# Third pair normalised in place, and a shorter way from the last token chunk to the first expert tile

## The reference

```python
mag = np.sqrt(a_re * a_re + a_im * a_im)
scale = np.minimum(mag, 0.999) / (mag + 1e-06)
a_re_n, a_im_n = (a_re * scale, a_im * scale)
for t in range(S):                                   # 768 steps
    new_re = ar * S_re - ai * S_im                   # state D x D, D = 48
    new_im = ar * S_im + ai * S_re
    S_re, S_im = (new_re + outer(k[t], v[t]), new_im)
    y[t] = q[t] @ S_re
```

```python
logits = xn @ en.T / tau
expert_idx = np.argmax(logits, axis=1)
for e in range(E):
    mask = expert_idx == e
    out[mask] = gate_w[mask, None] * (np.maximum(x[mask] @ w1[e], 0.0) @ w2[e])
```

## Time and profile before

| | |
|---|---|
| median of 3 runs | 994.85 us (993.94 to 995.58) |
| the profiled execution, its own time | 994.46 us |
| its span | 992.7 us |
| PE (TensorE matmul) busy | 872.8 us, 88% |
| DVE (VectorE) busy | 658.2 us, 66% |
| POOL (GpSimd) busy | 495.0 us, 50% |
| ACT (ScalarE) busy | 462.5 us, 47% |

### The profile page before, as it was taken

One profiled execution on the slowest core, in us unless ns is written; L12 is line 12 of the kernel. 1 busy time (PEld: TensorE's weight loads), 2 busy tenths in 40 slices (PEclk: granted clock), 3 DMA queues, 4 the chain that ended last, 5 costly groups with the idle time before them and its releaser, 6 DMA issues.

```text
span 992.7 us, 18419 instructions
## 1 busy us (share of the span) xinstructions
PE 872.8 (88%) x6398; PEld 776.7 (78%) x6399; DVE 658.2 (66%) x1054; ACT 462.5 (47%) x859; POOL 495.0 (50%) x888
## 2 busy tenths in 40 slices
PE   1658888788989998999999999839999999999995
PEld 1446777687879888889889888838888888888785
DVE  5967876789798998999876755167323252556722
ACT  4776734555646566565344441133222242446521
POOL 1291999699977978889791000023222232323221
PEclk9968997999999999999999999967999999999998
DMA  9104241352424243231311110334411141406311
GB/s 303 62 19 124 79 118 38 77 138 83 113 68 103 69 122 92 82 85 55 86 60 42 38 45 19 138 137 159 175 39 41 40 167 40 166 32 210 122 40 32
DMA packets 42247, 90.80 MB, mean 91 GB/s; under 512 B 6312, under 2 KB 23728, under 8 KB 40768
## 3 DMA queue, kind: packets, MB, share of 16 engines
q1 hardware_dynamic: 38080, 77.48, 25.7%
q0 software_dynamic: 4096, 12.40, 4.0%
HBM read 70.20 MB, written 18.48 MB: 89 GB/s over the span
## 4 chain that ended last, share of the span: by engine, by line
PE 55%; DVE 19%; issue 8%; ACT 8%; DMA 4%; POOL 4%; SPq 1%; DVEq 0%; ACTq 0%; POOLq 0%
PE mm L1582 7%; PE mm L1586 6%; PE mm L1583 6%; PE yu L1582 4%; PE tr L1582 4%; PE tr L1586 4%; PE tr L1583 4%; PE yu L1583 4%; PE yu L1586 4%; PE mm L1820 3%; PE sc L1639 2%; DVE l_im L1094 2%; DVE l_re L1093 2%; PE yu L1680 2%; DVE h_sb L1113 1%
## 5 line engine op out<-in xcount | busy, mean ns | idle before, releaser
L1582 PE MATMUL mm<-up_hi,x_hi 128*128 128x384 f32 x432 | 160.1, 371 | 41.0 <-DVE h_sb L1113 28.9
L1583 PE MATMUL mm<-up_lo,x_hi 128*128 128x384 f32 x432 | 150.7, 349 | 0.0
L1900 POOL TENSOR_TENSOR c_re<-ring 112x128 f32<-112x128 f32 x165 | 99.0, 600 | 102.2 <-DMA ring<-an_scratch 54.0
L1582 PEld LDWEIGHTS mm<-up_hi,x_hi 128*128 128x128 f32 x432 | 83.5, 193 | 57.1 <-DVE h_sb L1113 32.4
L1978 POOL DMA_INDIRECT out_rows<-g_o,rows_out x30 | 34.6, 1155 | 181.7 <-DVE g_o L1499 181.7
L1901 POOL TENSOR_TENSOR c_im<-ring 112x128 f32<-112x128 f32 x165 | 117.9, 714 | 0.0
L956 ACT ACTIVATE g_h<-tr 128x512 f32<-128x512 f32 x60 | 35.9, 598 | 171.2 <-PE tr L1586 165.7
L1586 PE MATMUL mm<-up_hi,x_lo 128*128 128x384 f32 x432 | 103.8, 350 | 0.0
L1904 POOL TENSOR_TENSOR ring<-c_re,c_im 112x64 f32<-112x64 f32 x165 | 91.7, 556 | 0.0
L1903 POOL TENSOR_TENSOR ring<-c_re,c_im 112x64 f32<-112x64 f32 x165 | 80.3, 487 | 12.9
L1113 DVE TENSOR_TENSOR h_sb<-mm,h_sb 128x384 f32<-128x384 f32 x96 | 53.0, 552 | 49.8 <-PE mm L1586 47.9
(11 more groups left out here) (242 smaller groups left out, 2091.4 us busy)
## 6 DMA issues: line engine op xcount, KB each, us to landing
raw<-in_moe_w SPq DMA_DIRECT2D x16, 1536.0 KB
a_dn<-in_a_laid SPq DMA_DIRECT2D x20, 384.0 KB, 6.9
an_scratch<-a_dn SPq DMA_DIRECT2D x20, 384.0 KB, 2.3
ring<-an_scratch SPq DMA_DIRECT2D x20, 384.0 KB, 5.5
q_in<-in_q_laid SPq DMA_DIRECT2D x24, 224.0 KB, 3.0
k_in<-in_k_laid SPq DMA_DIRECT2D x24, 224.0 KB, 3.1
v_in<-in_v_laid SPq DMA_DIRECT2D x24, 192.0 KB, 3.3
x_scratch<-x_sb SPq DMA_DIRECT2D x24, 192.0 KB, 2.1
```

What stands on the lines that cost most here:

```text
L1582: nc.tensor.matmul(out, hi[:, x, :], w_hi(x), start=(x == 0), stop=False)
L1583: nc.tensor.matmul(out, hi[:, x, :], w_lo(x), start=False, stop=False)
L1900: nc.gpsimd.tensor_tensor(c_re[:, 0:count, :, :], cur, bc(prev[:, :, 0, :], 2, 2), ALU.mult).then_inc(chain_prod, 1)
```

## The change

It has two groups of edits.

In the loop: `DIRECT` becomes 3, so pair 2 (units 4 and 5) is loaded straight into `ring` and normalised there, and its two stores and its read back are gone; units 6 to 9 are loaded at the start. The joins of pair 3 move: one behind the decay in turn 4, two early in turn 5, where `stage_z` now stands late. `norm_mag` of a turn's first unit moves ahead of `moe_out` and of `z_recip` on ScalarE, and `norm_sum` of its second unit moves behind `z_newton` and a `moe_max` on VectorE. In `moe_out` the copy of the router columns comes first.

In the routing: VectorE no longer waits for the last store of the tokens, and begins when the last router columns are there. The steps that only the gates need move behind the one-hot matrices, on all engines. The constants are written by GpSimd two chunks sooner (they get memory of their own for it). `row_hot` of the first six chunks is written ahead of `token_hot`. `gate_hot` moves from GpSimd to VectorE. VectorE writes the row lists of the first two gathers itself. The 24 steps of the gates' product (`gates`) move on TensorE between the first and the second matrix of the first tile, and what VectorE makes of them (`tables`) into the first tile. ScalarE starts to split expert 0 two pieces sooner, without the wait for the stores.

```diff
-DIRECT = 2
+DIRECT = 3
...
         joins_early = {1: [(1, b) for b in range(NBLK - 1)]}
         joins_late = {}
         joins_late[2] = [(2, 0)]
         joins_early[3] = [(2, 1), (2, 2)]
-        for g in range(3, NG):
+        joins_late[4] = [(3, 0)]
+        joins_early[5] = [(3, 1), (3, 2)]
+        for g in range(4, NG):
...
+            load_first(4)
+            load_first(5)
...
-                    store_unit(4)
-                    store_unit(5)
                 if n in ring_at:
                     load_ring(ring_at[n])
-                if n == 0:
-                    load_unit(8)
-                    load_unit(9)
...
+                nc.scalar.activation(z_all[:, at, :].rearrange("p t e -> p (t e)"), mm[:, 1, HD:NX], ACT.Copy) \
+                    .then_inc(x2_taken, 1)
...
-                late_z = n in (1, 3)
+                late_z = n in (1, 3, 5)
...
                     norm_rsqrt(4, norm_of(4))
                 if prev:
                     moe_copy(n - 1, 0)
+                for m in norms[:1]:
+                    norm_mag(m, norm_of(m))
                 if prev2:
...
-                for m in norms:
+                for m in norms[1:]:
...
-            act.wait_ge(x2_stored, 16 * NC)
-            for n in range(PIECES):
+            split_hi(0, 0, 0)
+            split_hi(0, 0, 1)
+            act.wait_ge(route_dve, 2)
+            nc.scalar.activation(r_tmp[:, :, :], logit[:, :, :], ACT.Exp).then_inc(route_act, 1)
+            for n in range(2, PIECES):
...
-                for m in norms:
+                for m in norms[:1]:
                     norm_sum(m, norm_of(m))
                 if more:
                     z_newton(n + 1)
                 if prev:
                     moe_max(n - 1, 0, 2)
+                for m in norms[1:]:
+                    norm_sum(m, norm_of(m))
...
-            dve.wait_ge(x2_taken, 2 * NC)
-            dve.wait_ge(x2_stored, 16 * NC)
-            nc.vector.tensor_scalar(nrm[:, 0, :], ssq_all[:, :], TINY, None, ALU.max).then_inc(route_dve, 1)
+            dve.wait_ge(x2_taken, 2 * NC - 1)
...
-            dve.wait_ge(route_act, 2)
-
-            squared = step(nc.vector.tensor_tensor(nrm[:, 3, :], nrm[:, 2, :], nrm[:, 2, :], ALU.mult))
+            dve.wait_ge(x2_taken, 2 * NC)
+            nc.vector.tensor_scalar(nrm[:, 0, :], ssq_all[:, :], TINY, None, ALU.max).then_inc(route_dve, 1)
             after(preferred)
             found = step(nc.vector.tensor_reduce(first[:, :], pick[:, :, :], AX.X, ALU.max))
-            after(squared)
-            newton = step(nc.vector.scalar_tensor_tensor(nrm[:, 4, :], nrm[:, 0, :], -0.5, nrm[:, 3, :], ALU.mult, ALU.mult))
             after(found)
             nc.vector.tensor_tensor(hot[:, :, :].rearrange("p e t -> p t e"), pick[:, :, :], bc(first[:, :], 2, E), ALU.is_equal) \
                 .then_inc(hot_made, 1)
+            dve.wait_ge(route_act, 2)
+            squared = step(nc.vector.tensor_tensor(nrm[:, 3, :], nrm[:, 2, :], nrm[:, 2, :], ALU.mult))
+            after(squared)
+            newton = step(nc.vector.scalar_tensor_tensor(nrm[:, 4, :], nrm[:, 0, :], -0.5, nrm[:, 3, :], ALU.mult, ALU.mult))
...
+            within = step(nc.vector.scalar_tensor_tensor(dest_at[:, 2, :], dest_at[:, 1, :], -float(P), dest[:, :], ALU.mult, ALU.add))
+
             nc.vector.tensor_tensor(in_slot[:, :, :], bc(dest_at[:, 1, :], 2, SLOTS), bc(slot_no[:, :], 1, NC), ALU.is_equal) \
                 .then_inc(in_slots, 1)
+            after(within)
+            nc.vector.tensor_tensor(row_hot[:, 0:CB, :], bc(dest_at[:, 2, 0:CB], 2, P), bc(row_no[:, :], 1, CB), ALU.is_equal).then_inc(rows_hot, 1)
             dve.wait_ge(in_slots, 1)
             nc.vector.tensor_tensor(token_hot[:, :, :], in_slot[:, :, :], bc(token_no[:, :], 2, SLOTS), ALU.mult) \
                 .then_inc(tokens_hot, 1)
-            for part in range(0, NC, CB):
+            for part in range(CB, NC, CB):
                 nc.vector.tensor_tensor(row_hot[:, part:part + CB, :], bc(dest_at[:, 2, part:part + CB], 2, P),
                                         bc(row_no[:, :], 1, CB), ALU.is_equal).then_inc(rows_hot, 1)
 
+            dve.wait_ge(route_act, 3)
+            total = step(nc.vector.tensor_reduce(gate[:, 0, :], r_tmp[:, :, :], AX.X, ALU.add))
+            step(nc.vector.tensor_copy(tiles_i[:, 0, :], bounds[:, 0:E]))
+            after(total)
+            guarded = step(nc.vector.tensor_scalar(gate[:, 1, :], gate[:, 0, :], 1e-9, None, ALU.add))
+            nc.vector.tensor_copy(tiles_i[:, 1, :], bounds[:, 1:E + 1]).then_inc(tiles_ready, 1)
+            after(guarded)
+            gated = step(nc.vector.reciprocal(gate[:, 0, :], gate[:, 1, :]))
+            after(gated)
+            high = step(nc.vector.tensor_copy(gate_parts[:, 0, :], gate[:, 0, :]))
+
             dve.wait_ge(rows_filled, 1)
+            for x in range(2):
+                nc.vector.tensor_scalar(rows_in[x][:, :], yb[:, x:x + 1], float(N // 2), None, ALU.add).then_inc(rows_ready, 1)
             nc.vector.tensor_scalar(fetch[:, :], yb[:, 0:SLOTS], float(N // 2), None, ALU.add).then_inc(fetch_ready, 1)
+
+            after(high)
+            low_part = step(nc.vector.tensor_tensor(gate_parts[:, 1, :], gate[:, 0, :], gate_parts[:, 0, :].bitcast(F32), ALU.subtract))
+            after(low_part)
+            for x in range(2):
+                nc.vector.tensor_tensor(gate_hot[:, :, x, :], in_slot[:, :, :], bc(gate_parts[:, x, :].bitcast(F32), 2, SLOTS), ALU.mult) \
+                    .then_inc(gates_hot, 1)
...
+            def tables():
+
+                dve.wait_ge(gates_filled, 1)
+                after(step(nc.vector.tensor_copy(row_gate[:, :, :], sc[:, 1, 0:2 * SLOTS].rearrange("p (x j) -> p x j", x=2))))
+                spare = step(nc.vector.scalar_tensor_tensor(spare_at[:, :], row_gate[:, 0, :], 0.0, spare_no[:, :], ALU.is_le, ALU.mult))
+                nc.vector.tensor_tensor(table_gate[:, :], row_gate[:, 0, :], row_gate[:, 1, :], ALU.add).then_inc(table_made, 1)
+                after(spare)
+                nc.vector.scalar_tensor_tensor(table_id[:, :], yb[:, 0:SLOTS], float(N // 2), spare_at[:, :], ALU.add, ALU.add) \
+                    .then_inc(table_made, 1)
+
+            def expert_tile(t, split=None, very_first=False):
                 gx_move(t + 1)
+                if very_first:
+                    tables()
...
+            def gates():
+                pe.wait_ge(gates_hot, 2)
+                for t in range(NC):
+                    last = nc.tensor.matmul(sc[:, 1, 0:2 * SLOTS], row_hot[:, t, :], gate_hot[:, t, :, :].rearrange("p x j -> p (x j)"),
+                                            start=(t == 0), stop=(t == NC - 1))
+                last.then_inc(gates_filled, 1)
...
+                if very_first:
+                    gates()
...
-            for g in range(DIRECT + 1, NG):
+            for g in range(3, NG):
...
-            pool.wait_ge(x2_taken, 2 * NC)
+            pool.wait_ge(z_staged, 3 * NC)
...
-            pool.wait_ge(in_slots, 1)
-            for x in range(2):
-                nc.gpsimd.tensor_tensor(gate_hot[:, :, x, :], in_slot[:, :, :], bc(gate_parts[:, x, :].bitcast(F32), 2, SLOTS), ALU.mult) \
-                    .then_inc(gates_hot, 1)
...
+            def gather(x):
+                pool.indirect_dma_start(g_in[:, x, :], None, x2_dram,
+                                        bass.IndirectOffsetOnAxis(ap=rows_in[x][:, :].bitcast(U32), axis=0)) \
+                    .then_inc(g_fetched[x], 16)
...
+            for x in range(2):
+                pool.wait_ge(rows_ready, x + 1)
+                gather(x)
             pool.wait_ge(fetch_ready, 1)
-            for x in range(2):
-                fetch_tile(x, x)
             pass_on(0, 0, 0)
+            pass_on(1, 0, 1)
             pool.wait_ge(table_made, 2)
             total = pool.value_load(tiles_i[0:1, 1, E - 1:E], min_val=E, max_val=SLOTS - 3)
-            for x in range(2):
-                expert_tile(x, 0, x)
+            store_tile(0, 0, 0)
+            expert_tile(1, 0, 1)
             with pool.Fori(1, total // 2) as pair:
                 for x in range(2):
                     expert_tile(2 * pair + x, pair, x)
```

More of the change, by code:

```diff
@@ L158, in sb2 @@
             return phase2.enter_context(nc.sbuf_tensor(name, shape, dt))
+        prefer = sb2("prefer", [P, E])
+        carry = sb2("carry", [P, E, NC])
+        bounds = sb2("bounds", [P, E + 1])
+        row_no = sb2("row_no", [P, P])
+        slot_no = sb2("slot_no", [P, SLOTS])
+        token_no = sb2("token_no", [P, NC])
+        spare_no = sb2("spare_no", [P, SLOTS])
         raw_1 = sb2("raw_1", [P, 2, KX, F2])
@@ L181, in attention_moe_program @@
         tiles_f = sb2("tiles_f", [P, 2, E])
-        bounds = sb2("bounds", [P, E + 1])
         tiles_i = sb2("tiles_i", [P, 2, E], I32)
@@ L477, in norms_in, with times_used @@
             return tuple(m for m in range(first, first + count) if m < NORMS)
+        def times_used(m):
```

(44 more changed lines are left out.)

44 lines of the change are left out of this document (7 added, 37 removed).

## The result

The changed kernel took 976.26 us (median of 4 runs, 975.51 to 978.39) against 994.39 (992.91 to 995.58) for the kernel before beside it: ratio 0.9822 [0.9801, 0.9843]. The forecast was 979.0 with a range of 971 to 989.

The account below looks back on a forecast made before the run. It took TensorE as the floor of late turns, with VectorE's waits and late staging lengthening early turns, and 29.9 us of routing with little TensorE work. Terms summed to -16.0 from 994.46, giving 978.5, forecast as 979, range 971 to 989.

Parts of the forecast that it names:

- Pair 2, turn 2: Loop turn 2: GpSimd starts pair 2 sooner, so VectorE's 3.47 us join wait goes; -3.5 us, bounds 0 and -3.7.
- rival 2: Early turns: TensorE's clock stays up through shorter holes, 5 to 8 us more come back; 972 us, chance 0.12.
- Turns from 6: Every second loop turn, paced by VectorE, loses the `norm_mag` wait in `norm_sum`; -7.0 us, bounds -3 and -9.
- Rival 5: Loop: `norm_mag` ahead of `moe_out` overfills ScalarE's hole and delays TensorE, 19 us over all gains; 998 us, chance 0.05.
- (a): Routing start: VectorE begins after the router columns' copy, not behind the store; -3.2 us.
- (c): Routing from `in_slot` to `fetch`, 10.6 us before: TensorE may start 2.9 us behind `in_slot`, 8.3 in all; -2.3 us.
- (f): First expert tile: the 24 gate steps, formerly hidden in the gather, now on TensorE's path; +2.65 us.
- (d): Routing from `fetch` to the gather: one VectorE instruction replaces GpSimd's copy, 0.35 instead of 1.66 us; -1.3 us.
- (e): Routing behind the gather: VectorE's `gate_hot` and three `split_lo` hide the gather; `g_x` at 671.0 instead of 677.25, -6.2 us.
- Rival 3: Routing: the gather is starved behind VectorE's run of 5.6 us, `g_x` at 674.5; 982.5 us, chance 0.08.
- Rival 4: First expert tile: gates run at the low clock, adding 2.65 and 1.6 us; 983 us, chance 0.07.
- Rival 1: Loop: late staging makes turn 5 a full old turn 3 and eats gains, 8.5 us together; 987.5 us, chance 0.20.

Follow-up runs that it names:

- the second profile after: The changed kernel, unchanged, timed and profiled again beside two other kernels on the same chip: 977.27 us, ratio 0.9822.
- the best kernel: Changed kernel with joins of pair 3 as before, gates' product ahead of the first tile, square of unit 6 behind `y_copy` in turn 0: 971.19 us, ratio 0.9763.

## Why the prediction was right, step by step

The time lay 2.7 us under the forecast, well inside the range. What the change does was foreseen, but part of the closeness is luck: startup and turns 1, 4 and 5 came out 4.4 us worse than forecast and turns 2, 3, those from 6 on and the routing 6.5 us better, so that -16.0 met -18.0.

- *Startup* was mis-sized: +0.6 for +3.3. The third pair's wider shapes on ScalarE and VectorE cost up to 1.0 in turn 0 (I had counted steps ahead of the first scores, and not that ScalarE's queue up to `y_copy` sets turn 0), the late clock 1.3, and the first mask's 0.94 lies within what it moves from run to run (70.64 to 75.12 in kernels with the same startup).
- *Pair 2, turn 2*: the mechanism was right and is shown. It gave -5.0 for -3.5, beyond my bound of -3.7: the clock of that turn (0.93 to 1.00), which I had left out, came on top.
- *Turn 1*: -0.26 for -1.0, and in the second profile after nothing at all (32.83). The hole that I took out was hardly on its path; what ended the turn instead I did not follow up.
- *Turn 3*: -2.64 for -2.0; the clock went from 0.84 to 0.98, which is rival 2 in part. Of the two turns that rival 2 named the other, turn 4, got 1.1 us of TensorE's busy time back (25.09 to 24.00), but turn 5 fell to 0.93.
- *Turns 4 and 5*: +1.47 for +0.5, with each half smaller than said, -3.6 for -6.8 and +5.1 for +7.3, the latter below my bound of +5.5. Taking the moved joins for something that breaks even was the error of judgment: by themselves they cost 3.7 there, of which turns 6 and 7 give back 1.4 to 2.8.
- *Turns from 6*: the mechanism was right (`norm_mag` put back, they are 275.60), the size was not: -11.07 for -7.0 and for a bound of -9, and still -9.1 in the second profile after (267.05). I had priced VectorE's idle time. In turn 16, 24.63 to 21.89, VectorE has no idle time between its wait of 1.49 and the `moe_max` for which TensorE then stands idle 2.09 us. The clock fell at 478.9, right behind that hole, and the turn's clock was 0.93, with TensorE's busy time at 22.17 instead of 21.41: 0.8 of the 2.7 there is clock. With `norm_mag` put back turn 16 had a hole of 1.68 us and a clock of 1.00, and took 23.29: 1.4 more than after without any fall of the clock, so a hole is not always followed by one. Turn 6 went from 0.94 to 1.00. Rival 5 is false by the two waits above: ScalarE's hole took `norm_mag` in, and nothing behind it was pushed.
- *Routing*: -3.85 for -3.6, and (a), (c) and (f) by themselves as forecast. (d) was counted at 1.3 for the gather but is worth nothing at `g_x`, since VectorE's queue of `gate_hot` and three `split_lo` ends later; my own step (e) had the gather hidden, and with it (d) was no gain. It did no harm to the sum, which went by `g_x`.
- *Rival 3*, the starved gather: the two gathers took 1.31 and 1.64 us on GpSimd beside `gate_hot` and `split_lo`, and 0.98 with nothing beside them at 657.50. Further on, four gathers that start beside a `split_lo` took 1.83 to 1.89 us, and those beside `gh_lo`, one of whose two inputs lies in PSUM and not in SBUF, 1.00 to 1.01 (the two lines below). So gathers beside two-input operations with both inputs in SBUF are slower, by up to 0.9, but far from the 3.5 that the rival needed. No run varied this alone. The rows go against the hardest reading of the Trainium skill, "SBUF — State Buffer", section "Who interferes with whom". Its inference that two-input operations do not lock descriptor generation out agrees with these rows, which show a delay and no lock-out.

```profile
776.32 1.89 POOL L1973 DMA_INDIRECT g_in<-x_scratch,rows_in  x1 [0.83 <-POOL rows_in L1978]
...
678.14 1.01 POOL L1973 DMA_INDIRECT g_in<-x_scratch,rows_in  x1 [0.27 <-POOL rows_in L1978]
```

- *Rival 4* is false: the clock rose at 663.0, ahead of the gates, which took 2.76. My 683.3 for the rise in the kernel before was misread: a mean clock of 0.66 from 683.00 to 684.00 puts it at 683.7, 4.4 us behind the first matrix, which changes nothing in the sum.
- *Rival 1* is false in the main: turn 5 had 26.0, not above 31.

By halves, in turns 1 to 22 (523.75 us before, turn 0 and its clock left out): the third pair alone gave -0.4 (523.36), where my terms for it, -3.5, -0.5, -5.2 and +8.8, make -0.4; `norm_mag` and `norm_sum` alone gave -13.8 (509.96), where my terms make -12.6; the two together gave -16.6 on average over the six profiles with both and no further edit of the loop (506.26 to 508.83). Some 2.4 us thus exist only in company: once `norm_mag` is in time, VectorE waits 5.94 and not 3.47 for pair 2, and there is more for the third pair to take away. The 2.4 is a difference of single profiles, and the six with both lie 2.6 apart.

What stays open is why the clock rises early or late in turn 0, what the joins' move costs over the whole loop, and whether the 6 us of the best kernel are all of its edits' making.

## What to carry to other kernels

An instruction that another engine waits for belongs into the nearest hole of its own queue, even ahead of work that looks more urgent: two instructions moved past seven on ScalarE (`moe_out`, `kp_copy` and `z_recip`) were worth nearly the whole loop's gain, while taking a pair's round trip through memory away showed no gain in time until that had been done and its companion edit left out. Price a wait with what stands behind it on the waiting engine and with the clock of the engine that idles in the end, not by its own length. When a change carries a companion edit (here the moved joins), try it without; and before a microsecond is explained, look at whether the same kernel shows it in another execution.
